# Layer two's first product for chunk pairs 0 and 1: from sixteen quarters to fourteen products, each over both pairs for one half of the tokens

## The reference, cut to what matters

```python
# attention: 2 batches, 8 heads, 768 positions, head size 64; 4 sinks and a window of 128
x = attention(q, k, v)                 # 1536 tokens x 512
h = x @ w_in                           # 1536 x 1024
e = exp(h - max(h)); solu = h * e / (sum(e) + 1e-9)
ln = (solu - mean) / sqrt(var + 1e-6) * g_ln
x2 = ln @ w_out                        # 1536 x 512
g = max(x2 @ w2_in, 0) ** 2            # 1536 x 2048: layer two's first product
out = g @ w2_out                       # 1536 x 512
```

## Time and profile before

| | |
|---|---|
| Median of 3 runs | 470.56 us (470.23 to 470.58) |
| The profiled execution: its own time | 471.22 us |
| Its span in the trace | 469.4 us |
| TensorE busy | 459.4 us, 98% |
| DVE, ACT, GpSimd busy | 75%, 50%, 27% |
| Chain that ended last: TensorE's share | 87% |

### The profile page before, as it was taken

How to read it: one execution, slowest core, us unless ns; L and a number is a source line. 1 busy time by engine, 2 the same in 40 slices (tenths; PEclk the granted TensorE clock), 3 DMA queues, 4 the chain that set the end, 5 groups by cost and what they waited for, 6 DMA issues and landing times.

```text
span 469.4 us, 8094 instructions
## 1 busy us (share of the span) xinstructions
PE 459.4 (98%) x2970; PEld 403.1 (86%) x2970; DVE 352.7 (75%) x592; ACT 236.3 (50%) x605; POOL 125.9 (27%) x175
## 2 busy tenths in 40 slices
PE   8989999999999999999999999999999999999997
PEld 6657787787778888788999999999988899888997
DVE  2899889988898898975682666666799997442792
ACT  3678777756765765644362222213545355222450
POOL 2356333051302311522245765553000000000000
PEclk9999999999999999999999999999999999999999
DMA  7921234543654773565401110111520011100011
GB/s 224 323 67 56 67 68 137 168 122 82 172 156 106 187 183 98 137 138 132 109 17 47 45 34 13 46 45 46 182 88 0 1 47 45 46 0 1 22 46 68
DMA packets 61471, 41.92 MB, mean 89 GB/s; under 512 B 28344, under 2 KB 50104, under 8 KB 61432
## 3 DMA queue, kind: packets, MB, share of 16 engines
q1 hardware_dynamic: 60664, 40.74, 31.2%
q10 hardware_dynamic: 768, 0.66, 0.5%
HBM read 30.38 MB, written 11.01 MB: 88 GB/s over the span
## 4 chain that ended last, share of the span: by engine, by line
PE 87%; DVE 4%; POOL 3%; DMA 2%; ACT 1%; issue 1%; SPq 1%; POOLq 0%; DVEq 0%
PE h_ps L1959 11%; PE wo_ps L1999 11%; PE wo_ps L2245 7%; PE score_ps L2161 7%; PE h_ps L2193 5%; PE score_ps L2193 5%; PE score_ps L2214 5%; PE wt_ps L2214 5%; PE h_ps L2214 5%; PE wo_ps L2193 4%; PE wt_ps L2193 4%; PE wo_ps L1921 3%; PE score_ps L1887 2%; PE wt_ps L2245 2%; PE score_ps L2245 2%; PE wo_ps L2024 2%
## 5 line engine op out<-in xcount | busy, mean ns | idle before, releaser
L1220 ACT ACTIVATE ring<-g 128x512 fp32r<-128x512 f32 x66 | 40.8, 630 | 50.8 <-PE h_ps L2214 12.0
L1673 DVE TENSOR_TENSOR g_low<-g,ring 128x512 fp32r<-128x512 f32 x66 | 45.0, 690 | 27.6 <-ACT ring L1220 26.9
L956 ACT ACTIVATE prob<-sm,nbias 128x132 f32<-128x132 f32 (+1 forms) x96 | 37.7, 394 | 4.7 <-DVE nbias L1334 4.0
L1959 PE MATMUL h_ps<-w_hi,xT_hi 128*128 128x512 f32 x88 | 35.2, 401 | 1.2 <-DVE xT_lo L1443 0.9
L1999 PE MATMUL wo_ps<-wo_hi,lnT_hi 128*128 128x512 f32 x88 | 36.1, 411 | 0.0
L2245 PE MATMUL wo_ps<-wst,ring 128*128 128x256 f32 x192 | 35.3, 283 | 0.0
L1999 PE MATMUL wo_ps<-wo_hi,lnT_lo 128*128 128x512 f32 x88 | 34.9, 397 | 0.0
L1999 PE MATMUL wo_ps<-wo_lo,lnT_hi 128*128 128x512 f32 x88 | 34.4, 391 | 0.0
L1959 PE MATMUL h_ps<-w_hi,xT_lo 128*128 128x512 f32 x88 | 34.4, 391 | 0.0
L1959 PE MATMUL h_ps<-w_lo,xT_hi 128*128 128x512 f32 x88 | 34.3, 390 | 0.0
L879 POOL TENSOR_TENSOR w_lo<-w_raw,w_hi 128x512 fp32r<-128x512 f32 x16 | 22.1, 1384 | 41.9 <-ACT w_hi L1184 41.9
(11 more groups left out here) (250 smaller groups left out, 1382.3 us busy)
## 6 DMA issues: line engine op xcount, KB each, us to landing
u_dram<-uT SPq DMA_DIRECT2D x18, 256.0 KB, 3.3
lnT_raw<-u_dram SPq DMA_DIRECT2D x36, 128.0 KB, 2.9
w_raw<-w_in SPq DMA_DIRECT2D x16, 256.0 KB, 3.3
V<-v SPq DMA_DIRECT2D x12, 256.0 KB, 3.3
x_dram<-x SPq DMA_DIRECT2D x44, 64.0 KB, 2.2
out<-y SPq DMA_DIRECT2D x11, 256.0 KB, 2.0
k_raw<-kT SPq DMA_DIRECT2D x20, 132.0 KB, 2.8
q_raw<-qT SPq DMA_DIRECT2D x20, 128.0 KB, 2.8
```

What stands on the lines that cost most here:

```text
L956: nc.scalar.activation(prob[:, h, seen(n)], sm[:, h, seen(n)], ACT.Exp, bias=nbias[:, h:h + 1], scale=-1.0 if alone(n) else SCALE, accum_o ...
L1220: nc.scalar.activation(item_high(n), item_raw(g, n), ACT.Copy).then_inc(item_rounded, 1)
L1673: nc.vector.tensor_tensor(item_raw(g_low, n), item_raw(g, n), item_high(n).bitcast(F32), ALU.subtract).then_inc(item_split, 1)
L1959: done = mm(h_ps[:, cols], xs[:, c, :], ws[:, c, cols], start=(c == 0 and k == 0), stop=(c == MC - 1 and k == 2))
```

## The change

Pairs 0 and 1 are multiplied by the seven products too. One product (`block_product(m, n)`) covers both pairs for one token half m: pair 0 and pair 1 in the two banks of one PSUM pair, two chunks, three pairs of hi and lo, twelve matmuls. So there are fourteen products, 168 matmuls, for sixteen quarters, 192. Two stand ahead of tile 10's projection, one between the transposes of tile 11 and its projection, eleven behind.

What goes with it: pair 1's w2 is loaded right behind pair 0's (into a buffer of its own), and pairs 2 and 3 ahead of x2T's third piece, each waiting for splits on GpSimd. GpSimd makes the sums for pairs 0 and 1; its sums and last parts lie where the hi of T1 and the hi and lo of T4 go later, so these two are rounded only when all eight early splits are done. x's B12 is no longer rounded or split; T1 to T4 of each half are made earlier. ACT keeps three copies and DVE makes four corner adds per token half (PSUM plus g), in place of sixteen copies on ACT. Four gates of 128x1536 (one a row and half, over both pairs) follow in pairs 2 to 5. The first items wait for the gates through pair 6.

The core of the diff:

```diff
+BLOCK_PRODUCTS = ((A11, B11, 0, True), (A12, B21, 1, True), (S2, T2, 0, False), (S1, T1, 1, True),
+                  (S3, T3, 0, False), (A22, T4, 2, True), (S4, B22, 1, False))
+M_FIRST, M_SECOND, M_SIXTH, M_FIFTH, M_SEVENTH, M_FOURTH, M_THIRD = range(NP)
+CORNERS = ((0, 0), (1, 1), (1, 0), (0, 1))
+GATES = tuple((m, r) for m in range(PASSES) for r in (1, 0))
+EARLY_PARTS = ((0, 0), (1, 0), (0, 1), (1, 1), (0, 2), (0, 3), (1, 2), (1, 3))
...
                 if since(j, 2):
-                    sp.wait_ge(w2_split, w2_parts_before(j - 1))
+                    sp.wait_ge(w2_split, w2_parts_until(j - 2, 3))
                 for r in range(2):
                     cols = slice((r * NJ + j) * P, (r * NJ + j + 1) * P)
...
                 if t == NT - 3:
                     load_w2(0)
+                    load_w2(1)
             load_x2T(1, TPB, TPB + QH3, x2T_loaded[1])
             store_x2(NT - 3)
             sp.wait_ge(lnT_split, len(LN_PARTS) * (NT - 1))
-            load_w2(1)
+            store_x2(NT - 2)
             load_w2(2)
-            store_x2(NT - 2)
+            load_w2(3)
             load_x2T(1, TPB + QH3, NT - 1, x2T_loaded[2])
             store_x2(NT - 1)
             load_x2T(1, NT - 1, NT, x2T_end_loaded)
...
-            split_w2(0)
+            split_w2(0, 0)
+            sum_w2_upper(0)
+            split_w2(1, 0)
+            sum_w2_upper(1)
+            sum_w2_lower(0)
+            sum_w2_lower(1)
             inverse_std(NT - 1)
-            split_w2(1)
+            for j, part in EARLY_PARTS[CLASSIC:]:
+                split_w2(j, part)
...
-                if k == T4:
-                    act.wait_ge(multiplied, len(QUARTERS) * CLASSIC * (s + 1))
+                if s == 0 and k in (T1, T4):
+                    act.wait_ge(w2_split, w2_parts_before(CLASSIC))
+                elif s == 1 and k in (T2, T3):
+                    for read in (B21, B22, T3):
+                        act.wait_ge(xc_split[0][read], 1)
                 nc.scalar.activation(x_hi(s, k)[:, :, :], x_combination(s, k), ACT.Copy).then_inc(xc_rounded[s][k], 1)
...
-                    act.wait_ge(g_ready, gates_before(PLAIN))
+                    act.wait_ge(g_ready, gates_before(NJ - 1))
...
             round_x(0, B21)
-            round_w2(0)
+            round_w2(0, 0)
+            round_w2(1, 0)
+            round_w2(0, 1)
             hidden_exp(NT - 1)
             hidden_sum(NT - 1)
-            round_x(0, B12)
             for part in range(len(LN_PARTS)):
                 round_lnT(NT - 2, part)
-            drain(0)
+            keep_first(0)
+            round_w2(1, 1)
+            round_x(0, T2)
             round_x(0, B22)
-            drain(1)
-            round_w2(1)
+            for j, part in EARLY_PARTS[2 * CLASSIC:]:
+                round_w2(j, part)
...
+            def add_corner(m, i):
+
+                r, h = CORNERS[i]
+                product, bank, added_to = ((M_SECOND, 1, (1, 0)), (M_FIFTH, 1, (1, 0)), (M_FOURTH, 2, (1, 0)), (M_THIRD, 1, (0, 1)))[i]
+                dve.wait_ge(multiplied, multiplied_before(m) + product + 1)
+                dve.wait_ge(block_kept, 3 * m + (1, 3, 3, 2)[i])
+                if i == 2:
+                    dve.wait_ge(block_added, len(CORNERS) * m + 2)
+                nc.vector.tensor_tensor(block_corner(m, r, h), block_pair(m, bank), block_corner(m, *added_to), ALU.add
+                                        ).then_inc(block_added, 1)
...
+            def block_product(m, n):
+
+                wk, xk, bank, opens = BLOCK_PRODUCTS[n]
+                pe.wait_ge(xc_split[m][xk], 1)
+                if n == M_FIRST and m == 0:
+                    pe.wait_ge(merged, merges(NT))
+                elif n == M_SECOND and m == 1:
+                    pe.wait_ge(block_added, 3)
+                elif n == M_SIXTH:
+                    pe.wait_ge(block_kept, 3 * m + 1)
+                elif n == M_FIFTH:
+                    pe.wait_ge(block_added, len(CORNERS) * m + 1)
+                elif n == M_SEVENTH:
+                    pe.wait_ge(block_kept, 3 * m + 2)
+                elif n == M_FOURTH and m == 0:
+                    pe.wait_ge(x2_squared, NT)
+                elif n == M_FOURTH:
+                    pe.wait_ge(block_kept, 3)
+                elif n == M_THIRD:
+                    pe.wait_ge(block_added, len(CORNERS) * m + 2)
+                for j in range(CLASSIC):
+                    if m == 0:
+                        pe.wait_ge(w2_split, w2_parts_until(j, (0, 0, 1, 1, 2, 2, 3)[n]))
+                    for c in range(2):
+                        for k in range(3):
+                            ws, xs = ((w2_hi, xc_hi), (w2_hi, xc_lo), (w2_lo, xc_hi))[k]
+                            last = mm(block_pairs[m][bank][:, j, 0:TH], ws[j][:, wk, c, :], xs[m][xk][:, c, :],
+                                      start=(opens and c == 0 and k == 0), stop=(c == 1 and k == 2), skip_group_check=True)
+                last.then_inc(multiplied, 1)
             def multiply(j, n):
...
-            pe.wait_ge(merged, merges(NT))
-            quarter(0)
-            quarter(1)
+            block_product(0, M_FIRST)
+            block_product(0, M_SECOND)
             project(NT - 2, 0, 24)
             transpose_ln(NT - 1)
-            quarter(2)
+            block_product(0, M_SIXTH)
             project(NT - 1, 0, 24)
-            for n in range(3, 16):
-                quarter(n)
+            for n in range(M_FIFTH, NP):
+                block_product(0, n)
```

216 lines of the change are left out of this document (111 added, 105 removed).

## The result

The changed kernel takes 473.73 us (median of 4 runs, 473.22 to 474.14); the kernel before, beside it, 470.57 (median of 4, 470.23 to 471.64). The ratio is 1.0063, with a 95% interval of 1.0047 to 1.0080. That is slower by 0.63%, three times the 0.2% named in the prediction.

The account below looks back on a forecast made before the run. TensorE was taken to bound the kernel, alone on the chain from 206.44 us to the last drain. Stalls of 4.7 us against 4.2 saved gave +0.5: median 471.1 us, range 468.2 to 473.8.

Parts of the forecast that it names:

- the slower rival: DVE row between tile 11's split and square, and half 1's T4 split: turns cost more, 472.8 to 474.5 us; chance 0.30.
- the case that I held likeliest: Whole kernel: 4.7 us lost against 4.2 saved, +0.5, median 471.1 us, own range 470.2 to 472.2; chance 0.45.
- Saved, 24 x 0.174 = 4.2 us: TensorE, pairs 0 and 1: 168 matmuls in place of 192, at 0.174 us each, save 4.2 us.
- Sixth product of half 0, 0.85: TensorE waits for T2's split, behind GpSimd's splits and the normalisation in turns: start 217.65 for 216.8, stall 0.85 us.
- the walk: Place-by-place pricing of stalls on TensorE from the first product to pair 2 and later; 4.7 us lost.
- Projection of tile 11, 0.4: ACT does five rounds before tile 11's transposes, from 219.2: projection starts 220.15 for 219.75, stall 0.4 us.
- Third product of half 0, 0.35: x2T load issued at 223.9, landing 4.76 us later, then rounds, corner copy, splits and add: 232.25 for 231.9, stall 0.35 us.
- Sixth product of half 1, 2.6: Half 1's sums wait for tile 11's round trip through memory: start 241.0 to 241.2 for 238.5, stall 2.6 us.
- Fourth product of half 1, 0.5: T4's split is last of five DVE operations, with one GpSimd split of pair 2 in turn: stall 0.5 us.
- Sum: Whole kernel: 0.85 + 0.4 + 0.35 + 2.6 + 0.5 = 4.7 us lost, 4.2 saved: +0.5.
- all is hidden: Rival, whole kernel: nothing lost, 466.4 us, needing half 1's sums by 236; chance 0.05.
- The signs the prediction named: New profile: DVE's last-square transpose near 228.5, x2T_second's last landing near 237, 2 to 3 us gap ahead of the tenth product.

Follow-up runs that it names:

- trial 5: Changed kernel, with w2's parts (0, 1) and (1, 1) split on GpSimd ahead of tile 11's variance, not behind it; the median shows no gain.
- trial 1: Changed kernel, with the loads of w2's pairs 2 and 3 behind both last x2T loads on SP's queue; the time is the same.
- trial 9: Changed kernel, with only the load of w2's pair 3 behind the last two x2T loads; no gain in the median.
- Trial 2: Changed kernel, with half 0's third-product corner copied and summed ahead of half 1's B11 and B21 roundings and splits; median 473.90 us.
- trial 6: Changed kernel, with half 1's B22 and T4 rounded ahead of pair 2's first w2 part; gain of 0.9 to 1.2 us, trial 12 included.
- trial 12: The edit of trial 6 on the changed kernel once more, for a profile at full clock; medians of both 0.9 and 1.2 us below the changed kernel's.
- trial 3: Changed kernel, with tile 11's squares ahead of half 0's T3 and T4 splits; median 1.3 us lower, executions in groups of mean 471.88 and 474.32 us.
- trial 7: Changed kernel with the edits of trials 2, 3, 6 and 9 together; 0.37% faster than the kernel before.
- trial 11: Trial 7, with GpSimd's splits of (0, 1) and (1, 1) after T2 and corner sum (0, 3) behind half 1's T1 and T2; both medians 468.65 and 468.66 us.
- trial 8: Changed kernel with the edits of trials 2, 3 and 6 together; 4.6 us faster than the changed kernel, 0.33% faster than the kernel before.
- trial 10: Trial 2's order, with half 1's second product made twice to fill TensorE's wait; median 472.67 us.

## Why the prediction missed the size

The median came out at 473.73 us, 2.6 above the 471.1 forecast and 0.07 inside the range's upper end of 473.8. That it fell inside is luck. The verdict, slower, had the largest chance (0.40), but 0.30 of that was the slower rival's, and the case that I held likeliest was a loss of 0.5 us. By its own steps:

- **Saved, 24 x 0.174 = 4.2 us**: right. TensorE is busy 3.7 us less by the page, and the products keep 2.08 to 2.09.
- **Sixth product of half 0, 0.85**: 0.47. The mechanism was right (the normalisation in turns with two splits, trial 5). Two splits and the normalisation took 3.0 us together (211.30 to 214.31) where the walk had 3.44 for them.
- **Projection of tile 11, 0.4**: nothing. ScalarE came to its five roundings 0.6 sooner, behind T2's, and they took 2.4 us, not 2.6; it rounded the transposes from 218.36, not 219.2.
- **Third product of half 0, 0.35: this is the step whose mechanism failed**, 2.84. "The x2T load goes out at 223.9 instead of 221.00 and lands 4.76 later as before": it went out sooner, at 223.10, and took 7.2 us. I had taken the time from issue to use from a queue on which the last issues of w2 ended 7.6 us ahead of it (at 213.44, for 221.00), when here 1 MB of w2 had been issued in the 2.7 us ahead. Trials 1 and 9 give 5.2 us with no load of w2 just ahead and 5.5 with half. Of the 2.5 us too few, 1.7 are the product's later start (233.94 for 232.25) and 0.8 that TensorE came to it sooner (231.10 for 231.9), from the two places above. Trial 2 shows the second half of the same step: even so late, the load costs this product nothing if the copy and the sum that don't need it go first.
- **Sixth product of half 1, 2.6**: 0.79. Half 1's sums began when the walk said (data at 237.1; T1 at 237.17), and TensorE started at 241.04, inside the forecast 241.0 to 241.2. In part that is luck, since T1 stood behind a corner's sum that waited for the third product, and not behind the load alone. The wait is small only since TensorE was already late from the third product. Together the two places were forecast at 2.95 and cost 3.63. The squares were done 1.0 to 1.3 us sooner than forecast (227.52), but from their store's first issue to T1 it took 9.6 us, not 8.4, of which some tenths may be that corner's sum.
- **Fourth product of half 1, 0.5: the term that made the sum too small**, 1.57. TensorE started the sixth product of this half as forecast (241.04), so the third product's long wait had cost nothing beyond the forecast by then, and all of the block's miss lies behind: 1.1 us here and some 0.2 in the starts behind the waits. This is the slower rival's mechanism, at the place it named: "GpSimd's second split of pair 2 comes ahead of DVE's split of T4, and that place alone goes from 0.5 to 1.9". Trials 6 and 12 remove it by order alone. The rival was right in this one place. Its general claim, that every operation is 0.04 to 0.07 us longer, was not needed: the walk's other turns came out shorter than forecast.
- **Sum**: 4.7 lost forecast, 6.0 measured. That makes +1.9 and not +0.5 in the block. The forecast median is 2.7 too low by parts: 1.3 in the span, 0.2 outside it, and 1.2 because the kernel before was profiled 0.66 above its median and the changed one 0.51 below its own. The first is the walk's; the last is how executions differ, the clock included.
- **What had no term**: the clock. No wait of 2 to 3 us stood in TensorE's chain before, so the page of before had nothing to show of it. In half of the changed kernel's runs it adds 0.7 us, and in trial 3 2.4. And the time outside the span rose from 1.8 us to 2.0 (471.22 less 469.4; 473.22 less 471.2), in every trial 2.0 to 2.1; why was not tried.
- **The rivals**: "all is hidden" needed the sums of half 1 by 236; trials 7 and 11 have T1 at 234.2 and 234.0, and still keep 1.4 to 1.7 us of waits. The full gain of 4.2 us was not reached by any order tried; 2.4 us of it (45.23 to 42.88) was.

The signs the prediction named: the squares near 228.5 were at 226.82, the landing near 237 held, and its own test said that if the largest gap stood elsewhere than at half 1's sixth product the walk was wrong. It stood at half 0's third.

## What to carry to other kernels

When the time from issue to use of a DMA is taken from a trace, look at what had been issued on that queue in the microseconds ahead of it, there and in the new order; a load on the way to the next wait belongs ahead of weights that are due 20 us later. On an in-order engine, put what a waiting engine needs next ahead of what needs a late load, whatever half of the work it belongs to. And if one removed wait gives nothing, don't drop the edit before the waits behind it are removed too: edits worth 0, 0, 1.3 and 1 us alone gave 5 together (3.7 of them in the traced stretch). Ask, too, which wait still costs time at the end: with the largest one here, 2.84 us, nearly gone, the next product that had to wait for data started only 0.5 to 0.6 us sooner after the first product (trials 1 and 9).

## What the runs showed that had not been expected

- A wait of TensorE for data brings its granted clock down for the matmuls behind it, but not in every execution. The changed kernel and trials 1, 2, 3, 5, 6, 9 and 12, whose longest wait is 1.9 to 4.0 us, had a mean clock below 0.998 in 36 of 55 executions; trials 7, 8, 10 and 11, whose longest is 0.8 to 1.6, in 3 of 39. The price: 3.42 + 2.56 us for two products in place of 2.33 + 2.08 in trial 3's trace, and 2.4 us between its two groups of executions. The kernel before, with no such wait, had the lower value in 2 of 59.
- Two executions can differ by 2 us before the changed part is reached: the first product started at 205.0 to 207.0 us in twelve traces. A change of half a microsecond was to be seen only in the stretch from the first product to pair 2's, as between trials 7 and 11 (43.36 and 42.88), not in medians of nine runs. Even there a trace is one execution: from tile 11's load's first issue to T1 it took 5.6 us in trial 2's and 4.3 in trial 10's.
